# Routing and expert network in one program: the first tiles of experts 0 and 1 run while the last tokens are routed

## What is computed

```python
def _moe_ref(x, w_in, w_out):                 # x: 3072 x 384, w_in: 384 x 2048, w_out: 2048 x 384
    h = x @ w_in
    g = np.where(h > 0.0, h, np.exp(np.minimum(h, 0.0)) - 1.0)
    return g @ w_out

def _moe2_ref(x, w_gate, w_noise, noise, w1, w2):   # E = 8, w1: 8 x 384 x 1024, w2: 8 x 1024 x 384
    noisy_logits = x @ w_gate + np.log1p(np.exp(x @ w_noise)) * noise
    top2 = np.argpartition(-noisy_logits, 2, axis=1)[:, :2]
    ...                                       # softmax over the two chosen scores gives top2_w
    for e in range(E):
        for k in range(2):
            mask = top2[:, k] == e
            h = np.maximum(x[mask] @ w1[e], 0.0)
            out[mask] += top2_w[mask, k, None] * (h @ w2[e])
```

## Time and profile before

| | us |
|---|---|
| median of 3 runs | 1310.47 |
| lowest, highest | 1308.33, 1697.81 |
| profiled execution, its time | 1309.26 |
| profiled execution, its span | 1307.5 |
| what lies around the span | 1.76 |

### The profile page before, as it was taken

The page is one execution under the profiler, slowest core; times in us unless marked ns, Lnnn a source line. Parts: engine busy times, 40 slices in busy tenths (PEclk is TensorE's granted clock), DMA queues, the critical chain, the costliest instruction groups (busy, mean ns, idle before and its releaser), DMA issues. The chain is left out here.

```text
span 1307.5 us, 29642 instructions
## 1 busy us (share of the span) xinstructions
PE 1133.8 (87%) x11688; PEld 1066.2 (82%) x11689; DVE 671.1 (51%) x1552; ACT 458.5 (35%) x992; POOL 340.0 (26%) x322
## 2 busy tenths in 40 slices
PE   4438798897799999999999960999999999999991
PEld 3326676676799999999999950999999999999991
DVE  6886756654445464655646524535444353544321
ACT  1124454565343334334343322423333242333220
POOL 4297792054000200101001012112222221222212
PEclk9968999999899999999999985999999999999996
DMA  5602434841910101101011951444342525222221
GB/s 119 149 23 63 120 87 104 286 102 26 367 39 1 56 13 44 55 0 55 12 43 66 330 171 56 133 136 120 77 135 43 137 42 138 50 48 43 41 43 24
DMA packets 75636, 117.52 MB, mean 90 GB/s; under 512 B 10970, under 2 KB 67066, under 8 KB 74010
## 3 DMA queue, kind: packets, MB, share of 16 engines
q1 hardware_dynamic: 59354, 77.14, 20.5%
q0 software_dynamic: 15040, 20.14, 8.6%
q10 hardware_dynamic: 1152, 19.00, 3.8%
HBM read 70.38 MB, written 45.93 MB: 89 GB/s over the span
## 5 line engine op out<-in xcount | busy, mean ns | idle before, releaser
L1615 PE MATMUL ps_yd<-hg,w_parts 128*128 128x400 f32 x1152 | 235.2, 350 | 0.0
L1013 PE MATMUL ps_h<-xr,w_parts 128*128 128x384 f32 x1152 | 224.0, 339 | 9.7 <-DVE xr L1164 9.3
L1598 PE MATMUL ps_hd<-xg,w_parts 128*128 128x400 f32 x1152 | 226.7, 345 | 1.3 <-DVE xg L1517 1.3
L1024 PE MATMUL ps_x<-w_parts,act_r 128*128 128x384 f32 x1152 | 218.0, 334 | 0.0
L1013 PEld LDWEIGHTS ps_h<-xr,w_parts 128*128 128x128 f32 x1152 | 201.8, 189 | 15.5 <-issue 14.0
L1598 PEld LDWEIGHTS ps_hd<-xg,w_parts 128*128 128x128 f32 x1152 | 211.4, 189 | 1.8 <-issue 1.6
L1440 POOL DMA_INDIRECT out_dram<-y_rows,token_now x68 | 107.8, 1585 | 383.3 <-issue 237.8
L1615 PEld LDWEIGHTS ps_yd<-hg,w_parts 128*128 128x128 f32 x1152 | 205.3, 188 | 0.0
L1024 PEld LDWEIGHTS ps_x<-w_parts,act_r 128*128 128x128 f32 x1152 | 201.3, 188 | 0.2 <-DVE act_r L1176 0.2
L1540 DVE SCALAR_TENSOR_TENSOR hg<-ps_hd,hg 128x400 fp32r<-128x400 f32 x128 | 73.5, 575 | 247.0 <-ACT hg L1478 247.0
L991 POOL DMA_INDIRECT xs_scratch<-x,rows_now x48 | 51.5, 1073 | 422.3 <-DVE rows_now L1257 254.1
(11 more groups left out here) (167 smaller groups left out, 1256.5 us busy)
## 6 DMA issues: line engine op xcount, KB each, us to landing
xs_scratch<-pads SPq DMA_DIRECT2D x8, 1965.0 KB, 17.7
x_rows<-xs_scratch SPq DMA_DIRECT2D x17, 614.1 KB
kqT<-in_kqT_dram SPq DMA_DIRECT2D x48, 192.0 KB, 3.9
carried<-in_w_dram ACTq DMA_DIRECT2D x3, 3072.0 KB, 10.7
w_raw<-in_w_dram ACTq DMA_DIRECT2D x3, 3072.0 KB, 11.9
inversion<-in_w_io_dram SPq DMA_DIRECT2D x4, 1536.0 KB, 12.5
out_dram<-pads SPq DMA_DIRECT2D x1, 4800.0 KB, 31.5
xt_scratch<-yT SPq DMA_DIRECT2D x48, 96.0 KB, 2.2
```

Of the source, the lines that this page charges most:

```text
L1013: mm = nc.tensor.matmul(ps_h[f % 2][:, 0:TB], wi[:, a, k, f * P:(f + 1) * P], xr[:, b, k, :], start=(i == 0), stop=(i == len(passes) - 1))
L1024: mm = nc.tensor.matmul(ps_x[t][:, 0:D], act_r[:, f % RING, a, t * P:(t + 1) * P], wo[:, b, f, :], start=(f == 0 and i == 0), stop=(f == F ...
L1598: mm = nc.tensor.matmul(ps_h[f % 2][:, 0:TR], w1r[i][:, a, k, f * P:(f + 1) * P], xg[:, b, k, :], start=(m == 0), stop=(m == len(passes) - 1))
L1615: mm = nc.tensor.matmul(ps_y[k][:, 0:TR], w2r[i][:, a, s, k * P:(k + 1) * P], hg[:, s % RING, b, :], start=(s == 0 and m == 0), stop=(s == ...
```

## The change

- **One block.** The two functions become one, `elu_network_and_experts`. The barrier between them goes, and so do the setting of dummy values, and the waits of SP at the end of the first block. PSUM banks and several on-chip tensors are shared by both networks (`ps_t, ps_y = ps_r, ps_x`; `xr` is a part of `xg`, `act_r` of `hg`, `x2T` of `yT`).
- **First tiles made final.** After the routing of block 6 (of 0 to 7), the next free row of experts 0 and 1 is raised to at least `TR` (`least`). So rows 0 to 399 of these regions are final before the last block is routed. If the expert has 400 rows or more by then, raising changes nothing; otherwise pad rows stand in the gap.
- **Order of tiles.** Expert 0's first tile, expert 1's first tile, expert 0's later tiles, expert 1's later tiles, then experts 2 to 7 as before. The first `turn` stands in block 7's last steps, and the routing of block 7 is spread over the steps of the first tile by three tables of its own (`TENSOR_LAST`, `SCALAR_LAST`, `VECTOR_LAST`).
- **Pads.** SP writes `LEAST` = 896 pad rows at the start of every region early in the ELU network, before the first scatter, and `PAD` = 512 rows behind each region's rows once the last block is scattered. All tiles from the third one on are loaded after that.
- **Own weights.** The first tile of expert e splits its own weights as it goes (`own`): the first two chunks ahead of it (`round_ahead`, `split_ahead`), the others one step or two ahead of their use. Raw weights of expert e+2 are loaded behind expert e's first tile.
- **Routing.** SCORE is made with tokens in partitions (nine products of 16 columns with the turned tokens as weights), so that BACK goes. PLACE sums the blocks of tokens in PSUM by four products instead of two, and VectorE has 5 steps there instead of 11. Routing stages stand up to two steps earlier.
- **Start.** SP waits for the first tokens before it issues the two weight loads.

```diff
-LATE = 2
-PAD = -(-(LATE * TB + TR) // P) * P
-REG = N - LATE * TB + PAD
+EARLY = 2
+LEAST = -(-2 * TR // P) * P
+PAD = -(-TR // P) * P
+REG = N + PAD
-TENSOR_STAGES = {1: TURN, 3: SCORE, 5: BACK, 11: PLACE}
-VECTOR_STAGES = {5: SOFT, 6: FIT, 7: REFINE, 8: TOP, 9: CHOOSE, 10: COLUMNS, 12: PLACE}
+TENSOR_STAGES = {1: TURN, 3: SCORE, 9: PLACE}
+VECTOR_STAGES = {3: SOFT, 4: FIT, 5: REFINE, 6: TOP, 7: CHOOSE, 8: COLUMNS, 10: PLACE}
+TENSOR_LAST = {1: TURN, 2: SCORE, 7: PLACE}
+VECTOR_LAST = {2: SOFT, 3: FIT, 4: REFINE, 5: TOP, 6: CHOOSE, 7: COLUMNS, 8: PLACE}
...
 # SP
+            for e in range(E):
+                pad(e * REG, LEAST, least_padded)
...
+            sp.wait_ge(rows_scattered, NX - TT * SLOTS * 16)
+            for e in range(EARLY):
+                load_rows(e, e * REG)          # waits for about_taken >= e + 1
             sp.wait_ge(counts_ready, 1)
-            sp.wait_ge(rows_scattered, NX - LATE * TT * SLOTS * 16)
+            sp.wait_ge(rows_scattered, NX)
             for e in range(E):
...
+                pad(rows + e * REG, PAD, pads_written)
             sp.wait_ge(pads_written, E * 16)
+            later_tiles(nc.sync, lambda e, lo: tile(e, lo, lo), tile)
...
 # GpSimd
+            with nc.gpsimd.Fori(0, NBK - 1) as r:
+                scatter(r)
+            pool.wait_ge(rows_loaded, EARLY * 16)
+            scatter(NBK - 1)
+            pool.wait_ge(out_cleared, 16)
+            pool.sem_inc(y_free, 2)
+            add_rows(0)
...
 # TensorE
+            def turn(t):
+                pe.wait_ge(rows_loaded, t * 16 + 16)
+                if isinstance(t, int) and t < 2:
+                    pe.wait_ge(rows_ready, NBK + t)
...
+            block_of_tokens(NBK - 1, True, then_turn=True)   # turn(0) ahead of the last second product
+            for e in range(EARLY):
+                expert_tile(e, e, True)
+            later_tiles(nc.tensor, first_tile, tile)
...
 # ScalarE, in the first tile of an expert: its own weights, step by step
+                    if own:
+                        if f < FTE - LAG:
+                            round_chunk(e, w1_chunk, f + LAG)
+                        round_chunk(e, w2_chunk, f)
+                    if own and e == 0:
+                        route_stage(NBK - 1, SCALAR_LAST.get(f))
...
+                if e + 2 < E:
+                    act.wait_ge(own_split, e * OWN + OWN)
+                    act.dma_start(w_raw[e % 2][:], w12[e + 2]).then_inc(expert_loaded[e % 2], 16)
...
 # VectorE
+                    if isinstance(r, int) and r == NBK - 2:
+                        nc.vector.tensor_tensor(base[:, 0:EARLY], base[:, 0:EARLY], least[:], ALU.max).then_inc(raised, 1)
...
+            split_x(NBK - 1)
+            block_of_tokens(NBK - 1, True)
+            dve.sem_inc(relu_split, 2)
+            dve.sem_inc(about_taken, 1)
...
+            split_ahead(0)
+            turn(0)
+            for e in range(EARLY):
+                first_tile(e, e)
+            later_tiles(nc.vector, first_tile, tile)
```

More of the change, by code:

```diff
@@ L965, in _, with tile @@
             sp.wait_ge(pads_written, E * 16)
-            sp.wait_ge(rows_scattered, NX)
-            sp.wait_ge(expert_loaded[1], 16)
-            sp.wait_ge(out_cleared, 16)
+            def tile(e, t, lo):
+                at = e * REG + (t - lo) * TR
+                load_rows(t, nc.s_assert_within(at, 0, E * REG - TR,
+                                                skip_runtime_bounds_check_because="a region has room for all tokens' rows and a tile more"))
+            later_tiles(nc.sync, lambda e, lo: tile(e, lo, lo), tile)
@@ L970, in _ @@
+            last = bound(nc.sync, E)
+            sp.wait_ge(about_taken, last + 1)
+            sp.dma_start(x_rows[:], xs_dram[0:TR, :].rearrange("(a p) d -> p a d", p=TP)).then_inc(rows_loaded, 16)
+            sp.wait_ge(rows_loaded, last * 16 + 16)
+            sp.sem_inc(passed, 1)
         @block.gpsimd
@@ L1535, in take_rows, with expert_tile @@
                                         ).then_inc(y_ready, 1)
-            def tile(j, i, t, splitting):
+            def expert_tile(e, t, own):
+                first_of_all = own and e == 0
                 for f in range(FTE):
@@ L1559, in _ @@
+            with nc.vector.Fori(2, NBK - 1) as n:
+                split_x(n)
+                block_of_tokens(n, True)
+            split_x(NBK - 1)
+            block_of_tokens(NBK - 1, True)
             dve.sem_inc(relu_split, 2)
             dve.sem_inc(about_taken, 1)
[L1561 to L1562 removed]
+            dve.sem_inc(about_ready, 1)
+            dve.sem_inc(y_ready, TRT)
+            split_ahead(0)
             turn(0)
[L1564 removed]
+            for e in range(EARLY):
+                first_tile(e, e)
```

632 lines of the change are left out of this document (294 added, 338 removed).

## The result

| | before | after |
|---|---|---|
| median, us | 1309.95 (4 runs) | 1294.41 (4 runs) |
| lowest, highest, us | 1308.33, 1697.81 | 1292.24, 1296.38 |
| span of the profiled execution, us | 1307.5 | 1294.3 |
| mean clock of TensorE, share | 0.955 | 0.968 |

The 1697.81 is one slow execution, which the ratio leaves out.

A forecast was written before the change was run, and what follows sets the result against it. Bound: TensorE, its winnable idle time being 52 us between block 7's last product and the experts' first. Third turn at 850.3 + 2.5 + 433.95 + 4.4 - 3.5 = 1287.7 span, 1289 us; 8-in-10 range 1267 to 1303.

The forecast's parts named there:

- the two stops: TensorE's waits for rows before the first and third tiles' turns: 5.8 and 17.4 us, each with a 2.5 us cold start.
- The first stop: Before the first tile's turn, TensorE waits 5.8 us for rows whose load needs `about_taken`, counted behind block 7; clock falls.
- The first tile with the routing: First expert tile with block 7's routing inside: 27.8 us from its first product until rows are placed, at 804.2.
- From scatter to pads: On the queues after block 7's routing: 2.8 us from the last scatter, 813.5, to SP's first pad, 816.3.
- The pads: Eight last pads ahead of the third tile's load: 27 us, landed at 843.3, bounds 836 and 851.
- the second stop: Before the third tile's turn, TensorE stands still 17.4 us because its rows' load stands behind all pads.
- Routing in the blocks: New routing products in blocks 1 to 7: 0.5 us gained a block, 3.5 us in seven; bounds loss 15, gain 10.
- Own weights: Splitting weights inside each expert's first tile costs 4.4 us: 2 ahead of expert 2, 2.4 in six others; bounds 0 and 10.
- Behind the third turn: From the third tile's turn to the end: cold start 2.5, fourteen tiles and tail 433.95, splitting of weights 4.4 us.
- pads in time: Rival at the third tile: pads land early enough, no wait or cold start there, 1269 us; chance 0.20, in time or nearly.
- Code that isn't there: Rival at every tile: jumps to code not yet run stall TensorE, 3.4 us for each of fourteen, 1336 us; chance 0.05.
- Adds late: Rival: first tile's adds, beside pads and weights, stop VectorE, then TensorE, 1300 to 1305 us; chance 0.10, shared with dear routing.

The follow-up runs named there:

- experiment 1: The changed kernel with VectorE's first count of `about_taken` moved ahead of block 7, so SP loads the first tile's rows earlier: 1286.84 us, ratio 0.984.
- experiment 2: The changed kernel with raw weights of experts 2 and 3 both loaded behind expert 1's first tile: 1284.30 us, ratio 0.981.
- experiment 6: The kernel before, two programs and barrier kept, with only the new routing (SCORE, PLACE, earlier stages): 1295.09 us, ratio 0.989.
- 4: The changed kernel with expert 0's last pad written first, then the third tile's rows loaded, then the other seven pads: 1284.75 us, ratio 0.982.
- experiment 7: The changed kernel with each expert's last pad written and waited for ahead of that expert's own later rows: 1279.66 us, ratio 0.976.
- experiment 8: The changed kernel with early first load, weights of experts 2 and 3 later, a pad for each expert and packed layout: 1280.37 us, ratio 0.977.
- experiment 9: The changed kernel with early first load, a pad for each expert, packed layout, weights of experts 2 and 3 loaded behind tiles 3 and 4: 1270.23 us, ratio 0.970.

## Why the prediction came out as it did

The direction, the two stops, and the size within 5.4 us were right (15.5 us won where 21 were forecast). Part of that closeness is luck, since two errors of 6.4 and 3.5 us on neighbouring steps went opposite ways. Step by step, with the times of after less the 2.7 us by which the attention ended later:

- **The first stop.** Predicted 5.8 us, measured 4.7, its cause shown by experiment 1. The clock fell as foreseen, to 0.50: 2.26 us for the turn.
- **The first tile with the routing.** From its first product to the rows placed I put 27.8 us; they took 27.84 (777.29 to 805.13). The wait of the second turn for `rows_ready` is 1.33.
- **From scatter to pads.** This is the step that was mis-sized: "From there to the first pad were 2.8 us". It took 9.2, 6.4 too little, since the weight load stood beside the scatter. I had the load in the sum, but as 3 us of DMA time on the pads, as if it could only slow what is moved, not hold back what has to be complete. Without it (experiment 2) the gap is 2.7.
- **The pads.** 23.5 us against 27. With the load paid for already this is the near end of the same step. Together with the load of rows (6.5 for 5.96) the second stop came to 19.6 instead of 17.4.
- **Routing in the blocks.** Predicted 3.5 us gained; from the first product to block 7's last second products 0.9 were measured, and 0.3 to 1.0 in the other runs of the single program. The term itself was right: in the kernel before the new routing gives 3.9 (experiment 6). What failed is that nothing else in a block was to change: groups of nine products take 0.01 to 0.02 us longer in the merged program. A cost that small times 256 groups is 3 to 4 us, and no row of before could show it.
- **Own weights.** 3.0 measured against 4.4; the gap ahead of expert 2 was 2.1 against 2, as foreseen. The waits for `own_split` at each tile didn't come.
- **Behind the third turn** I had 440.9 (2.5, 433.95, 4.4); it is 440.2.
- **Attention.** 2.7 us later in this execution. The other kernels, with the same code up to there, lie on both sides of the kernel before.

The sum of the span, 1287.7, with what was measured: the last scatter 1.3 us later (routing in the blocks, less the shorter first stop and a quicker scatter), the gap behind it +6.4, pads -3.5, the load +0.5, what follows -0.7, the attention +2.7. That is 1294.4; the span was 1294.3.

Of the rivals, pads in time was excluded by 23.5 us of pads. Code that isn't there was worth nothing: TensorE's list of waits has no wait by issue at a tile. Adds late didn't come in the change, where the second stop gave them 20 us, but did in three of its improved versions (4, 7 and 8). And one rival was missing: that the routing edit, which I took for 3.5 us, was by itself worth the whole gain in the old frame, since the pads' 51 us stood in the way of block 6's scatter and so of TURN, 9.5 us, which I had in the timeline and didn't follow back. The single program adds 2 us of the stretch to it (959.7 to 957.5), and 22 more once its two stops are gone (935.2 in experiment 9). The single program with the old routing wasn't run. There TURN doesn't stand in the way of the first tile, so the two gains need not add up in the other order, and 2 us is not the worth of the single program by itself.

**The mechanism behind three of the waits.** Scatter and adds are both slowed to about the end of a weight load beside them, at two different places (9.2 against 2.7 us; 16 against 5.7 with two loads, and with one 13.8 in experiment 7 and 12.4 in 9, 857.60 to 869.97). The page's list of queues (packets, MB, share) for the change, where q0 has the indirect DMAs, q10 ScalarE's weight loads and q1 SP's:

```profile
q1 hardware_dynamic: 60506, 78.75, 20.9%
q0 software_dynamic: 14336, 19.53, 8.1%
q10 hardware_dynamic: 1152, 19.00, 4.0%
```

By division a packet has 1.3 KB in q1, 1.36 KB in q0, and 16.5 KB in q10. What the turns of the queues make of this is told by the Trainium skill (DMA: Bandwidth & Descriptors, Queues, rings and completion order): a DMA engine goes round the queues that have work and changes after each packet. I had cited that rule for equal shares of time. With packets 12 times as large it gives something else, if the packets that the profile counts are those of the rule, which no run shows: 192 packets of a weight load are 12 turns for each of 16 engines, while the 768 rows of a scatter (the 48 scatters and 64 adds of the page have 12,544 rows in q0's 14,336 packets, so about one to a packet) are 48, so the load would be through long before. The scatter's row agrees: the first pad at 823.23 is 13.3 us behind the load's issue. For the add of 100 rows in experiment 8, some 7 for each DMA engine, an estimate by the same rule of the Trainium skill is 5 us more, at 0.7 us for a large packet (24 of them in the 17 us of the two loads); it was 10, so the rule explains half of that one. What is shown is that a weight load beside them holds them up (experiment 2 against the change and 9 against 8 move only the loads). That packet size is the cause, and not some precedence of the queue, was not tried.

## What to carry to other kernels

When a barrier goes, list what DMA has to be complete for the next wait, and keep large loads out of those moments; a load that only has to be there 50 us later should be issued behind them, not where its buffer comes free. Write and wait for only what the next step reads: eight pads ahead of one tile cost 20 us, one cost 2. And before a large edit is credited with its gain, make its small companion alone in the old kernel, and the large edit without it.

## What was not expected of the hardware

- A small indirect DMA beside large loads is not slowed in proportion: it landed only about when they were done. An add took about 16 us instead of 5.7 beside 6 MB at 400 GB/s, and 12.4 to 13.8 beside 3 MB; beside eight pads of small packets two took 9.7 and 10.6 (in the change, from 826.38 and from 836.11).
- Groups of nine identical products kept different distances, 1.560 and 1.579 us, in two programs with the same rows for them, 128 x 384 by 128 x 128. Another distance between the operands' parts moved 0.008 us from the first products to the second and left their sum as it was.
- The same attention code ended anywhere within 5.3 us (332.2 to 337.5) in the profiled executions of twelve kernels, which is a third of the effect that was studied. No kernel was profiled twice here, so whether the execution or the program makes the difference stays open.
